# Keys in blocks of 32, routing steps in another order, and one ReLU chunk ahead of the fourth output copy

## The reference

```python
scores = scale * q @ k.T                      # masked: window 32, or every 4th of 128
attn = softmax(scores) @ v                    # -> x, 2304 tokens x 512
e_idx = argmax(x @ w_gate)                    # one expert per token
gate_w, eom = softmax(x @ w_gate)[e_idx], sigmoid(x @ w_output_gate)
out[mask] = gate_w * eom[e] * (relu(x[mask] @ w1[e]) @ w2[e])   # per expert, 1024 wide
h = out @ w_in                                # 2048 wide
result = (max(h, 0) + log1p(exp(-abs(h)))) @ w_out
```

## Time and profile before

| | |
|---|---|
| median of 3 runs | 784.24 us (783.22 to 786.44) |
| the profiled execution, own time | 778.8 us |
| its span, first to last instruction | 776.9 us |
| mean granted TensorE clock | 0.985 of full speed |
| attention and token tiles | 0 to about 113 us |
| routing, up to the first slot product | about 113 to 139.7 us |
| slots | 139.7 to about 376 us |
| dense layers | about 376 us to the end |

### The profile page before, as it was taken

How to read it: one execution, slowest core, us unless ns; L and a number is a source line. 1 busy time by engine, 2 the same in 40 slices (tenths; PEclk the granted TensorE clock), 3 DMA queues, 4 the chain that set the end, 5 groups by cost and what they waited for, 6 DMA issues and landing times.

```text
span 776.9 us, 14654 instructions
## 1 busy us (share of the span) xinstructions
PE 743.6 (96%) x5180; PEld 679.0 (87%) x5181; DVE 403.0 (52%) x847; ACT 376.8 (49%) x946; POOL 231.1 (30%) x230
## 2 busy tenths in 40 slices
PE   6899973999999999999999999999999999999997
PEld 5688862899999999999999999899899899899896
DVE  4577877546656677676733433433343334334332
ACT  6677741345535565654733533443353344335333
POOL 5223313646655777774260100000010010001001
PEclk9999996999999999999999999999999999999999
DMA  9998524646645577764200100010010000001001
GB/s 210 220 215 217 190 83 142 208 138 215 201 142 166 186 227 245 213 200 140 82 2 0 42 0 0 0 40 0 0 40 0 0 27 14 0 0 40 0 0 40
DMA packets 30083, 75.53 MB, mean 97 GB/s; under 512 B 4368, under 2 KB 12576, under 8 KB 30048
## 3 DMA queue, kind: packets, MB, share of 16 engines
q1 hardware_dynamic: 23440, 54.30, 24.2%
q0 software_dynamic: 5744, 16.04, 7.0%
q10 hardware_dynamic: 864, 4.74, 1.5%
HBM read 65.61 MB, written 9.46 MB: 97 GB/s over the span
## 4 chain that ended last, share of the span: by engine, by line
PE 92%; DVE 4%; issue 2%; DMA 1%; ACT 0%; SPq 0%; POOL 0%; DVEq 0%; ACTq 0%
PE bank L636 13%; PE bank L638 13%; PE bank L637 13%; PE bank L660 9%; PE bank L662 9%; PE bank L658 9%; PE bank L649 4%; PE bank L651 4%; PE bank L650 4%; PE bank L526 3%; PE bank L552 3%; PE bank L537 3%; PE bank L569 2%; PE bank L622 1%; DMA k_sb<-kT 1%
## 5 line engine op out<-in xcount | busy, mean ns | idle before, releaser
L1281 DVE SCALAR_TENSOR_TENSOR g_sb<-bank,soft 128x384 f32<-128x384 f32 x96 | 53.5, 558 | 230.4 <-ACT soft L958 230.4
L954 ACT ACTIVATE soft<-bank 128x384 f32<-128x384 f32 x96 | 47.1, 491 | 210.3 <-PE bank L638 210.3
L492 POOL DMA_INDIRECT out<-y_sb,out_rows_i x18 | 17.3, 960 | 348.6 <-ACT y_sb L965 346.8
L1140 DVE TENSOR_TENSOR w_lo<-raw,w_hi 128x1024 fp32r<-128x1024 f32 x68 | 92.7, 1364 | 53.5 <-ACT w_hi L867 53.1
L636 PE MATMUL bank<-x_parts,w_hi 128*128 (+1 forms) x352 | 110.5, 314 | 0.7 <-issue 0.7
L638 PE MATMUL bank<-x_parts,w_lo 128*128 (+1 forms) x352 | 110.0, 313 | 0.0
L637 PE MATMUL bank<-x_parts,w_hi 128*128 (+1 forms) x352 | 110.0, 312 | 0.0
L867 ACT ACTIVATE w_hi<-raw 128x1024 fp32r<-128x1024 f32 x68 | 71.9, 1060 | 51.0 <-PE bank L651 48.1
L425 POOL TENSOR_SCALAR xs_sb<-landing 128x256 f32<-128x256 f32 x48 | 65.2, 1368 | 59.3 <-PE bank L622 59.3
L649 PE MATMUL bank<-h_hi,w_hi 128*128 128x384 f32 (+3 forms) x256 | 80.8, 316 | 0.9 <-DVE h_lo L1161 0.9
L651 PE MATMUL bank<-h_lo,w_hi 128*128 128x384 f32 (+3 forms) x256 | 77.7, 303 | 0.0
(11 more groups left out here) (191 smaller groups left out, 1689.9 us busy)
## 6 DMA issues: line engine op xcount, KB each, us to landing
raw<-we SPq DMA_DIRECT2D x64, 512.0 KB, 3.9
x_tokens<-x_sb ACTq DMA_DIRECT2D x6, 771.0 KB, 3.7
v_sb<-vw SPq DMA_DIRECT2D x12, 384.0 KB, 8.8
raw_m<-wm POOLq DMA_DIRECT2D x8, 512.0 KB, 5.5
raw<-wm SPq DMA_DIRECT2D x8, 512.0 KB, 3.5
q_sb<-qT SPq DMA_DIRECT2D x12, 256.0 KB, 5.8
k_sb<-kT SPq DMA_DIRECT2D x12, 256.0 KB, 7.7
v_sb<-vw SPq DMA_DIRECT2D x4, 576.0 KB, 13.9
```

The costliest lines, as they stand in the source:

```text
L1140: nc.vector.tensor_tensor(w_lo[:, r, :], raw[:, r, :], w_hi[:, r, :].bitcast(F32), ALU.subtract).then_inc(w_lo_done, 1)
```

## The change

The keys lie in blocks of 32 positions, with the four pairs side by side in a block, in HBM and in `k_sb`. A load is then one piece of 2048 bytes (3072 for the last load) in each partition, and a score product reads three runs of 32 columns. The very first load of keys is issued by ScalarE, ahead of its table load. In routing, `block_token` comes first and `place_onehot` follows in three parts of 6 tiles (`PART`), for each of which TensorE waits apart. The count matrix `lower` holds -1 where it held 0 and 0 where it held 1, so that one subtraction (1110) is left out. `used_i` is made and read while TensorE sums, the sources are rounded straight from PSUM, two of the three scalings move ahead of three other steps, and the zeroing products are 5 rounds after the sums and none later. At a slot's end, ReLU chunk 0 of the next slot stands ahead of the fourth output copy, and its low part ahead of the fourth clearing.

```diff
-        k_sb = [sb(early, f"k_sb{s}", [P, PAIRS, S]) for s in range(2)]
+        k_sb = [sb(early, f"k_sb{s}", [P, S // WINDOW, PAIRS, WINDOW]) for s in range(2)]
...
-                sp.dma_start(k_sb[m][:, :, QT * lo:QT * hi], kT[b][:, :, QT * lo:QT * hi]).then_inc(loaded, 16)
+                k_lo, k_hi = QT * lo // WINDOW, QT * hi // WINDOW
+                if (b, lo) != (0, 0):
+                    sp.dma_start(k_sb[m][:, k_lo:k_hi], kT[b][:, k_lo:k_hi]).then_inc(loaded, 16)
...
-            pool.wait_ge(ones_ready, 1)
-            step(nc.gpsimd.affine_select(out=lower[:, :], in_=ones[:, :], compare_op=ALU.is_gt, fill=0.0,
+            step(nc.gpsimd.memset(lower[:, :], 0.0))
+            step(nc.gpsimd.affine_select(out=lower[:, :], in_=lower[:, :], compare_op=ALU.is_gt, fill=-1.0,
...
-                                                k_sb[m][r, c, k0:k0 + KEYS], start=False, stop=(c == PAIRS - 1),
+                                                k_sb[m][r, k0 // WINDOW:(k0 + KEYS) // WINDOW, c, :], start=False, stop=(c == PAIRS - 1),
...
-                pe.wait_ge(block_tokens, 2)
                 for t in range(NT):
+                    if t % PART == 0:
+                        pe.wait_ge(block_tokens, 2 + t // PART)
...
-                    if j == TPS - 1:
-                        zero_outputs(1)
...
-                            zero_outputs(4)
+                            zero_outputs(5)
...
-                                    zero_outputs(1)
...
+            k_hi = QT * LOADS[0][1] // WINDOW
+            act.dma_start(k_sb[0][:, 0:k_hi], kT[0][:, 0:k_hi]).then_inc(qk_loaded[0][0], 16)
...
+            def hidden_hi(f):
+                nc.scalar.activation(h_hi[:, f % RING % HRING, :], h_ps[f % 2][:, 0:SLOT], ACT.Relu
+                                     ).then_inc(h_hi_done, 1)
+
             def slot_parts(slot, last):
                 if not last:
                     other = bass.ds(act.snap((slot + used + 1) % 2, min_val=0, max_val=1), 1)
 
                 def hidden(f):
                     act.wait_ge(g1_done, slot * FC1 + (f + 1))
-                    nc.scalar.activation(h_hi[:, f % RING % HRING, :], h_ps[f % 2][:, 0:SLOT], ACT.Relu
-                                         ).then_inc(h_hi_done, 1)
+                    hidden_hi(f)
...
+                    if k == KC - 1 and not last:
+
+                        act.wait_ge(g1_done, slot * FC1 + (FC1 + 1))
+                        hidden_hi(0)
...
-            step(V.tensor_tensor(flat(tot), flat(cum), tot_ps[:, 0:NT * E], ALU.subtract))
-            step(V.tensor_tensor(tot[:, :, :], tot[:, :, :], X["row"][:, :].unsqueeze(2).to_broadcast([P, E, NT]),
+            step(V.tensor_tensor(tot[:, :, :], cum[:, :, :], X["row"][:, :].unsqueeze(2).to_broadcast([P, E, NT]),
...
-            V.tensor_tensor(place_onehot[:, :, :], column_no[:, :, :],
-                            place[:, :].unsqueeze(1).to_broadcast([P, P, NT]), ALU.is_equal).then_inc(block_tokens, 1)
...
+            for first in range(0, NT, PART):
+                t = slice(first, first + PART)
+                V.tensor_tensor(place_onehot[:, :, t], column_no[:, :, t],
+                                place[:, t].unsqueeze(1).to_broadcast([P, P, PART]), ALU.is_equal
+                                ).then_inc(block_tokens, 1)
+            V.tensor_copy(used_i[:, :], X["ov_cum"][0:1, E - 1:E]).then_inc(sizes_ready, 1)
+            dve.wait_ge(sizes_ready, 1)
+            used = overflow_slots(dve)
+            first_half = bass.ds(dve.snap(used % 2, min_val=0, max_val=1), 1)
 
             dve.wait_ge(sources_summed, 1)
-            step(V.tensor_scalar(source[:, :], source_ps[:, 0:BLOCKS], float(MIDDLE_TOKEN), None, ALU.add))
-            V.tensor_copy(source_i[:, :], source[:, :]).then_inc(sources_ready, 1)
-            step(V.tensor_scalar(half_source_i[:, 0, :], source[:, :], 2.0, None, ALU.mult))
-            V.tensor_scalar(half_source_i[:, 1, :], source[:, :], 2.0, 1.0, ALU.mult, ALU.add
+            V.tensor_scalar(source_i[:, :], source_ps[:, 0:BLOCKS], float(MIDDLE_TOKEN), None, ALU.add
+                            ).then_inc(sources_ready, 1)
+            V.tensor_scalar(half_source_i[:, 0, :], source_ps[:, 0:BLOCKS], float(MIDDLE_TOKEN), 2.0, ALU.add, ALU.mult
                             ).then_inc(half_sources_ready, 1)
+            V.tensor_scalar(half_source_i[:, 1, :], source_ps[:, 0:BLOCKS], float(MIDDLE_TOKEN) + 0.5, 2.0,
+                            ALU.add, ALU.mult).then_inc(half_sources_ready, 1)
...
+                    if k == KC - 1:
+
+                        dve.wait_ge(h_hi_done, slot * FC1 + (FC1 + 1))
+                        hidden_lo(0)
...
+            for j in range(TPS - 1):
+                scale_first(j)
...
-            dve.wait_ge(sizes_ready, 2)
-            used = overflow_slots(dve)
-            first_half = bass.ds(dve.snap(used % 2, min_val=0, max_val=1), 1)
-            for j in range(TPS):
-                scale_first(j)
+            scale_first(TPS - 1)
...
+            dve.wait_ge(h_hi_done, 1)
+            hidden_lo(0)
...
-        a = arranged(a).reshape(B, PAIRS, 2, S, D)
-        return np.ascontiguousarray(a.transpose(0, 2, 4, 1, 3).reshape(B, P, PAIRS, S))
+        a = arranged(a).reshape(B, PAIRS, 2, S // WINDOW, WINDOW, D)
+        return np.ascontiguousarray(a.transpose(0, 2, 5, 3, 1, 4).reshape(B, P, S // WINDOW, PAIRS, WINDOW))
```

More of the change, by code:

```diff
@@ L68 @@
 TILES_STORED = 3
+PART = NT // 3
 GATES = ((0, 6), (6, 3), (9, 3), (12, 6))
@@ L168, in build @@
         block_token = sb(early, "block_token", [P, NT, BLOCKS], F16)
-        source = sb(early, "source", [P, BLOCKS])
         early.close()
@@ L208, in build @@
         y_ps = bank[4:7]
-        consts_step, masks_ready, identities_ready, consts_ready, wg_loaded, masks_zeroed, ones_ready, \
+        consts_step, masks_ready, identities_ready, consts_ready, wg_loaded, masks_zeroed, \
             indices_ready, indices_spread = map(sem, (
                 "consts_step", "masks_ready", "identities_ready", "consts_ready", "wg_loaded", "masks_zeroed",
-                "ones_ready", "indices_ready", "indices_spread"))
+                "indices_ready", "indices_spread"))
         qk_loaded = [[sem(f"qk_loaded{s}_{n}") for n in range(len(LOADS))] for s in range(2)]
@@ L447, in _ @@
                     in_offset=bass.IndirectOffsetOnAxis(ap=source_i[:, j:j + 1], axis=0)).then_inc(first_rows[j], 16)
-            pool.wait_ge(half_sources_ready, 1)
+            pool.wait_ge(half_sources_ready, 2)
             for h in range(2):
@@ L900, in slot_parts @@
                     f = half * RING
-                    hidden(f)
+                    if f:
+                        hidden(f)
                     weights(f + 3)
@@ L926, in _ @@
                                      ).then_inc(x_hi_done, 1)
+            act.wait_ge(g1_done, 1)
+            hidden_hi(0)
             with act.Fori(0, E - 1) as slot:
@@ L979, in _ @@
             nc.vector.memset(ones_b[:, :], 1.0)
-            nc.vector.memset(ones[:, :], 1.0).then_inc(ones_ready, 1)
+            nc.vector.memset(ones[:, :], 1.0)
             nc.vector.memset(kinds_i[:, :], UNUSED)
@@ L1152, in zero_y, with hidden_lo @@
                 nc.vector.memset(yT_ps[k][:, 0:SLOT], 0.0).then_inc(y_zeroed, 1)
+            def hidden_lo(f):
+                r = f % RING % HRING
+                nc.vector.scalar_tensor_tensor(h_lo[:, r, :], h_ps[f % 2][:, 0:SLOT], 0.0,
+                                               h_hi[:, r, :].bitcast(F32), ALU.max, ALU.subtract
+                                               ).then_inc(h_lo_done, 1)
             def slot_parts(slot, last):
@@ L1158, in hidden @@
                 def hidden(f):
-                    r = f % RING % HRING
                     dve.wait_ge(h_hi_done, slot * FC1 + (f + 1))
-                    nc.vector.scalar_tensor_tensor(h_lo[:, r, :], h_ps[f % 2][:, 0:SLOT], 0.0,
-                                                   h_hi[:, r, :].bitcast(F32), ALU.max, ALU.subtract
-                                                   ).then_inc(h_lo_done, 1)
+                    hidden_lo(f)
                 def weights(c):
@@ L1210, in _ @@
             step(V.tensor_scalar(SL["taken"][:, :], SL["taken"][:, :], 0.0, None, ALU.max))
-            V.tensor_copy(used_i[:, :], X["ov_cum"][0:1, E - 1:E]).then_inc(sizes_ready, 1)
             step(V.tensor_scalar(SL["kind"][:, :], SL["taken"][:, :], float(SIZES[1]), None, ALU.is_le))
```

## The result

The changed kernel takes 777.12 us (median of 5 runs, 775.72 to 779.93), the kernel before 783.77 us beside it. The ratio is 0.9927, with an interval of 0.9899 to 0.9955. That is 6.65 us, twice the 3.15 of the sum. The same kernel was measured twice more, on two chips: 0.9933 [0.9906, 0.9959] and 0.9955 [0.9937, 0.9973], which is 5.2 and 3.5 us by the ratio, where the first measurement has 5.7 by its ratio. The time lies within the range, but most of the gain comes from places where the prediction had put nothing.

What follows compares the result with a forecast made beforehand. The prediction took TensorE, busy 743.6 of 776.9 us, as the bound. Start 0.75, routing 1.7 and slots 0.7 sum to 3.15 us, taking the median 784.24 to 781.1; range 776 to 785.5, the forecast's own 779 to 783.5.

Steps and rivals of the forecast that it cites:

- First keys: Kernel start: first keys issued by ScalarE beside the queries let TensorE start earlier; 0.75 us gained, bounds 0.4 and 2.6.
- Key layout in later units: Later attention units: score products reading three runs of 32 columns change nothing; 0 us taken, up to 24 us lost.
- The gap at 30.8 us: Attention: TensorE's 2.64 us idle without a semaphore inside 16 products was expected to stay; no gain counted.
- the gap goes: Rival, attention: the 2.64 us stop and slow stretch behind it vanish, 4.3 us together, giving 776.8; chance 0.17.
- Count matrix 0.34: Routing on VectorE: leaving out the subtraction at line 1110 makes the sources earlier by some 0.34 us.
- sums 0.9 − 0.1: Routing: 12 of 18 sums run beside comparisons, cutting VectorE's wait by 0.9 us; comparing in three parts costs 0.1.
- rounding, 0.23: Routing: rounding the sources straight from PSUM saves one step, 0.23 us, before the gathers.
- Zeroing products: Routing: without later zeroing rounds, first slot product at 136.5, not 139.71; 3.2 us at equal clock, 1.7 with low clock.
- The clock holds into the slots: Rival, first slot products: the clock stays high, so 3.2 us gained in place of 1.7, giving 779.6; chance 0.13.
- Slots, 0.7 us: Slots of 224 columns: moving ReLU and low part ahead shrinks two `h_lo` waits (0.34, 0.52); 0.7 us, bounds 0 and 0.9.
- Score products pay for runs: Rival, attention: three-run reads slow the score products; at 0.25 us per unit, 9 us lost, giving 790.1; chance 0.07.
- 5.4 us carried between the profiled execution and the median: Whole kernel: the median, 784.24, is 5.4 us above the profiled execution; that difference was carried into the forecast.

## Why the prediction was right, and where it wasn't

The time is within the range, but more than half of the steps behind it failed or came to nothing, and that the number came out so near is in part luck. The routing term was too high by 1.7 us and the keys' too low by 2.8. The forecast's own range, 779 to 783.5, missed; the stated one reached down to 776 for the sake of a rival. By its own steps:

- **First keys, 0.75 us.** Size and sign hold for the start: over four traces with the old keys the first mask product is at 5.65 on average (5.12 to 6.16), over eight with both edits at 4.99. The third unit is earlier by 1.0 us (10.4 to 9.4). But the cause was not shown to be the step's. With ScalarE's issue alone the start was no earlier (6.18), with the layout alone it was at 4.25, one trace each. And the step looked at two loads only, where every later load comes sooner too.
- **Key layout in later units, nothing.** This is the first step that failed. It priced the layout by what the products read, which was right (0.88 us as before), and not by what it does to the transfers. With the old keys the ranks start at 114.1 on average (113.2 to 115.4), with the layout alone at 111.6, with ScalarE's issue alone at 111.0, with both at 109.7 (108.6 to 110.5). The single edits are one trace each, and among the eight the ranks alone move by 2 us with the start of the short scores (108.6 where it is 9.5, 109.2 to 109.8 where 12.4 to 12.8, 109.8 to 110.5 where 15.1 to 15.8), so the parts can't be split exactly. By the times each alone gives 0.8 to 0.9 us, not told from nothing. Together they give 3.5 us (0.9955). In the window of 10 to 20 us the rate was 218 to 255 GB/s with keys in pieces of 512 bytes and 267 in pieces of 2048 (DMA share 1.08 to 1.09 and 1.07), 279 with the one load issued by ScalarE, and 290 to 313 with both. The Trainium skill ("DMA: Bandwidth & Descriptors", Specifications) says that 512 bytes suffice for the full rate, which would have left these transfers as they were; the runs speak against it for this stretch, though mildly (255 and 267 are near). The Trainium skill ("Trainium Kernel Development and Optimization", Key Constraints) says that issuing from several engines saves the issue time alone; the runs speak against that too, with 279.
- **The gap at 30.8 us, left as it is.** The second that failed, and the rival "the gap goes" (0.17) took its place. It is present in all six traces without both key edits (0.99 to 2.64 us) and gone in the eight with them (0 to 0.17). It ends 1.4 to 1.7 us after a packet of 16 KB of instructions, and that packet starts at 27.6 to 30.7 us in the six and at 25.4 to 27.3 in the eight. That the packet is late because it must wait behind full queues is only argued; no row shows when it was asked for. The rival was priced at 4.3 us and 776.8, close to the 777.12 measured, but not for its reason: the six traces give 0.99 to 2.64 us for the stop, and the clock fell behind it only in the first of them, after the longest.
- **Count matrix 0.34, sums 0.9 − 0.1.** The edits did shorten VectorE's chain and TensorE didn't start earlier. The step took VectorE as what the sums wait for, since the earlier trace rows names it. It was the sequencer, busy until 118.0 with two branches, and moving the sums ahead of them gave 1.7 us. The rows before had it already: `block_token` was ready at 124.31, the sums started 0.67 us later, and the second branch ended at 124.8. These two terms are zero in this kernel. Of the sources only the **rounding, 0.23**, came: from sums to the first gather 2.70 us before, 2.47 after.
- **Zeroing products, 3.2 us at equal clock, 1.7 in all.** The direction held, the size didn't. Counted from the ranks, the third transposes came 1.6 us earlier and the first product 1.0 (1.8 and 1.3 by the means over seven traces with the old routing and four with the new). The rounds had also covered 2.2 us of TensorE's own branches and register steps between the last transposes and the first product, which are idle now: TensorE stands 2.24 us for no releaser until 131.86, though VectorE's first low part was ready at 130.9:

```profile
130.31 1.95 DVE L1166 TENSOR_TENSOR x_parts<-bank,x_parts 128x384 f32 x4 [0.27 <-issue]
```

  The low clock came as forecast, in all four traces of the new order with no rounds behind the transposes (spacing of the first products 0.32 us), and in none of the seven of the old one. Together: the 25th slot product comes 31.8 us after the ranks with the edits and 31.5 without. The term was 1.7 and measured nothing (1.0004).
- **The clock holds into the slots** (0.13): it didn't. Where I forced it to, with three rounds behind the transposes, it held, and cost as much as it gave.
- **Slots, 0.7 us.** Right in mechanism; it measured 0.9 to 1.0 (224.0 to 223.1, alike in all traces of the two slot orders with the turns as they were), so a little more than the two waits.
- **Score products pay for runs, a new gap, slow VectorE parts**: none came. The three parts took 1.49 us together, the sum had 1.45.
- **The level of the clock in the earlier trace rows.** The prediction called the scores of 1.55 us those of the low level. No granted clock shows that: the column reads 1.00 for 5 to 10 us. The sum doesn't use it.
- **5.4 us carried between the profiled execution and the median.** This is the dense stage: in some executions it is 5.2 to 6.1 us longer. TensorE stands for 2.7 to 4.2 us near 400 us, nearly all of it in stops with no semaphore behind them, and in four of the five traces that have them the granted clock is then 0.50 for 3.4 or 6.8 us. In the fifth, the changed kernel's first, it isn't. Standing time and clock together leave up to 1.0 us of the longer stage unaccounted. No packet of queue q8 falls into these stops. The longer stage is in five traces: the first of the changed kernel and all four on the second chip, of the kernel before, the changed one and two between. It is in none of the eight on the first and the third chip. The first profile of before had missed it, the first one of after had it. Without its 5.2 us the spans would differ by 7.6 and not by 2.4, beside 6.65 for the medians. It would also account for the 5.4 us, which I was right to carry over, as the stops meet both kernels. What they are stays open.

The sum of what was measured: keys 3.5 on one chip, slots 1.2 (0.9985, not told from nothing) and routing 0 on another, so 4.7 us, where the whole change gives 5.2 (0.9933) on the first of the two, and 3.5 to 5.7 over its three measurements.

What stays open is why the issue of a single load from ScalarE brings the eighth load of keys in at 32.3 us and not at 36 to 38.7. It is one trace, but the eight with both edits stand against the one with the layout alone in the same way (30.1 to 31.8 and 35.0). The layout in the one is the old one, and the one issue that SyncE saves takes 0.67 us, far less than the 4 to 6 us.

## What to carry to other kernels

A releaser that the profile names is the last semaphore, not the last thing: before shortening what an engine waits for, look at the waiting engine's own sequencer, and compare the time at which the releaser ended with the time at which the waiter started. A stop with no releaser can be checked against the DMA queue that carries instructions. Work off the critical path, like the zeroing rounds here, can cover branches and hold the clock, so taking it away wins less than its length. Where a stage runs with its DMA queues full, price a change of layout by its bytes per piece first, and by what the engine reads second.

## What the runs showed of the hardware

- With the DMA engines full (share 1.04 to 1.09, 10 to 20 us), the queues moved 267 GB/s with keys in pieces of 2048 bytes in place of 218 to 255 with pieces of 512, 279 with one load issued from another queue, and 290 to 313 with both.
- The two compare-branches of TensorE's sequencer ahead of the sums took 2.9 to 5.5 us the first time, with one 16 KB packet of instructions of about 1 us in each, and 0.21 us at most later on.
- TensorE stopped without a semaphore around 31 us for 0.99 to 2.64 us in six traces with slower loads, each time until 1.4 to 1.7 us after a 16 KB packet of instructions. Near 400 us it stood for 2.7 to 4.2 us in all four traces of one chip and in the first of the changed kernel, with no such packet.
- The same program takes 776 us on one chip and 783 on another, 0.9%, more than the change gives, and 5.2 to 6.1 us of it are the longer dense stage that all four traces of the slower chip have; kernels were compared only beside each other.
